# Head pairs whose scores are three fp32r products of halves: from the ninth pair on instead of the eleventh

## What is computed

```python
def _attn_ref(q, k, v, cap) -> np.ndarray:
    scale = 1.0 / np.sqrt(q.shape[-1])
    scores = scale * np.matmul(q, k.transpose(0, 1, 3, 2))
    scores = cap * np.tanh(scores / cap)
    ...
    attn = np.exp(scores)
    attn = attn / (np.sum(attn, axis=-1, keepdims=True) + 1e-09)
    return np.matmul(attn, v).astype(np.float32)

def _moe_ref(x, w_in, w_out, s, b) -> np.ndarray:
    h = x @ w_in
    r = np.maximum(h, 0.0)
    g = s * (r * r) + b
    return (g @ w_out).astype(np.float32)
```

## Time and profile before

| | |
|---|---|
| Median of 3 runs | 625.73 us (625.71 to 626.56) |
| The profiled execution's own time | 625.9 us |
| Span of the profile | 624.0 us |
| Busy PE, PEld, DVE, ACT, POOL | 617.2, 480.3, 330.9, 258.4, 46.3 us |
| Score products L352 (pairs 0 to 9) | 120 instructions, 64x448 |
| Score products L393 (pairs 10 to 23) | 252 instructions, 64x448 |
| Granted PE clock | 9 in all 40 slices of the page, mean 1.00 |

### The profile page before, as it was taken

The page is one execution under the profiler, slowest core; times in us unless marked ns, Lnnn a source line. Parts: engine busy times, 40 slices in busy tenths (PEclk is TensorE's granted clock), DMA queues, the critical chain, the costliest instruction groups (busy, mean ns, idle before and its releaser), DMA issues.

```text
span 624.0 us, 8174 instructions
## 1 busy us (share of the span) xinstructions
PE 617.2 (99%) x3206; PEld 480.3 (77%) x3206; DVE 330.9 (53%) x565; ACT 258.4 (41%) x272; POOL 46.3 (7%) x46
## 2 busy tenths in 40 slices
PE   7999999999999999999999999999999999999998
PEld 3335666777777777777779999999888888888997
DVE  4986999998677677677663332222411121111311
ACT  7885455656555555555413322222411121111220
POOL 0115724700000000000000000000000000000000
PEclk9999999999999999999999999999999999999999
DMA  8432245343222222231014112222522234111501
GB/s 289 143 117 61 87 155 157 108 130 94 72 92 87 76 88 91 71 92 58 29 60 148 59 51 58 70 78 75 175 79 59 66 112 125 48 42 33 165 2 64
DMA packets 31863, 57.17 MB, mean 92 GB/s; under 512 B 3536, under 2 KB 18000, under 8 KB 31824
## 3 DMA queue, kind: packets, MB, share of 16 engines
q1 hardware_dynamic: 31824, 56.64, 28.6%
HBM read 40.11 MB, written 16.52 MB: 91 GB/s over the span
## 4 chain that ended last, share of the span: by engine, by line
PE 95%; DVE 2%; DMA 1%; issue 1%; ACT 0%; SPq 0%; ACTq 0%; DVEq 0%
PE banks L480 13%; PE banks L482 13%; PE banks L481 13%; PE banks L497 12%; PE banks L496 12%; PE banks L498 12%; PE banks L438 8%; PE banks L393 5%; PE banks L352 3%; PE banks L450 2%; PE banks L418 1%; DMA work<-w_in 1%; PE banks L461 1%; DVE e_sum L725 0%; DVE w_lo L707 0%
## 5 line engine op out<-in xcount | busy, mean ns | idle before, releaser
L480 PE MATMUL banks<-x_hi,w_hi 128*128 128x448 f32 x384 | 142.9, 372 | 0.0
L482 PE MATMUL banks<-x_hi,w_lo 128*128 128x448 f32 x384 | 140.7, 366 | 0.0
L481 PE MATMUL banks<-x_lo,w_hi 128*128 128x448 f32 x384 | 140.6, 366 | 0.0
L497 PE MATMUL banks<-x_lo,w_hi 128*128 128x512 f32 (+2 forms) x384 | 139.4, 363 | 0.0
L498 PE MATMUL banks<-x_hi,w_lo 128*128 128x512 f32 (+2 forms) x384 | 139.4, 363 | 0.0
L496 PE MATMUL banks<-x_hi,w_hi 128*128 128x512 f32 (+2 forms) x384 | 139.4, 363 | 0.0
L813 DVE SCALAR_TENSOR_TENSOR x_lo<-e,beside,x_hi 128x512 fp32r<-128x512 f32 (+1 forms) x48 | 32.5, 683 | 115.5 <-ACT x_hi L641 115.5
L480 PEld LDWEIGHTS banks<-x_hi,w_hi 128*128 128x128 f32 x384 | 72.1, 188 | 15.0 <-issue 8.3
L641 ACT ACTIVATE x_hi<-e,beside 128x512 fp32r<-128x512 f32 (+1 forms) x48 | 31.7, 669 | 116.7 <-PE banks L498 116.7
L496 PEld LDWEIGHTS banks<-x_hi,w_hi 128*128 128x128 f32 x384 | 72.1, 188 | 9.0
L497 PEld LDWEIGHTS banks<-x_lo,w_hi 128*128 128x128 f32 x384 | 72.1, 188 | 8.9
(11 more groups left out here) (67 smaller groups left out, 550.0 us busy)
## 6 DMA issues: line engine op xcount, KB each, us to landing
hidden_scratch<-hidden_sb SPq DMA_DIRECT2D x48, 224.0 KB, 1.9
beside<-q_k SPq DMA_DIRECT2D x23, 448.0 KB, 4.0
e<-hidden_scratch SPq DMA_DIRECT2D x32, 256.0 KB, 2.7
e<-w_out SPq DMA_DIRECT2D x16, 384.0 KB, 3.1
work<-w_in SPq DMA_DIRECT2D x22, 256.0 KB, 5.5
v_sb<-v SPq DMA_DIRECT2D x24, 192.0 KB, 2.5
y_t<-beside SPq DMA_DIRECT2D x10, 256.0 KB, 2.1
e<-hidden_scratch SPq DMA_DIRECT2D x16, 160.0 KB, 2.2
```

What stands on the lines that cost most here:

```text
L480: nc.tensor.matmul(out, w_hi[:, j, w], x_hi[:, batch % 2, c, :], start=c == 0, stop=False)
L481: nc.tensor.matmul(out, w_hi[:, j, w], x_lo[:, batch % 2, c, :], start=False, stop=False)
L482: last = nc.tensor.matmul(out, w_lo[:, j, w], x_hi[:, batch % 2, c, :], start=False, stop=c == CT - 1)
L497: nc.tensor.matmul(out, w_hi[:, j, w], ring(x_lo, n), start=False, stop=False)
```

## The change

`SPLIT` goes from 2 * 6 - 2 = 10 to 6 + 2 = 8. Pairs 8 and 9 now take the split form.

```diff
-SPLIT = 2 * PAIRS - 2
+SPLIT = PAIRS + 2
```

## The result

The kernel after takes 627.45 us in the median of 15 runs (626.67 to 628.23), the kernel before, run beside it, 626.52 us (625.57 to 627.04). The ratio is 1.0018 with a 95% interval of 1.0011 to 1.0025: slower by 1.1 us, between 0.7 and 1.6. The forecast was 0.92 us more, the same sign and within the range. The executions shown ahead of the prediction (625.73 in the median) were among the shorter ones of before; over 15 runs its median is 626.5, so it is the forecast difference, 0.92, and not the forecast time of 626.65 that is held against the runs.

The account below looks back on a forecast made before the run. PE was taken to bound the kernel, with a DVE stretch without idle time delaying a load PE depends on. Terms -0.86, +0.77 and +1.01 gave +0.92 on 625.73, so 626.65 us; range 625.2 to 627.9 (8 in 10).

Parts of the forecast that it names:

- PE gains 0.86 us: Score blocks of pairs 8 and 9 on PE: the split form saves 0.43 us a pair, 0.86 us for two.
- The casts on ACT are free: Two new casts of 0.94 us fit ACT's idle time before tanh operations and cost nothing, 0.2 and 0.7 us to spare.
- First stall 0.77 us: PE at pair 8's first scores waits 0.77 us for the low half, whose DVE subtraction takes 2.18 us beside POOL.
- the later wait: PE's second stall, +1.01 us, at the tail scores of pairs 10 and 11, waiting for the tanh of pair 10.
- S = 1.55 us: S is the delay of DVE's square ahead of tile 5's store and pair 11's load; taken as 1.55, bounds 1.0 to 2.6.
- a walk through POOL's window: Stepping through DVE and POOL operations where they exclude each other; it cut the square's delay from 2.00 to 1.55 us.
- PE is later by S - 0.63: From the tail scores of pairs 10 and 11 on, PE lags by the square's delay less 0.63 us, whatever came earlier.
- Nothing behind the tail scores: After the tail scores of pairs 10 and 11 no further loss was counted: later loads are covered by ACT's and PE's slack.
- The term for the wait: At the tail scores of pairs 10 and 11, PE starts 0.1 us after the tanh it waits for ends.
- the sum: PE's total lateness at the tail scores of pairs 10 and 11: 1.55 - 0.63 = +0.92 us.
- The rival "slower": A square delay of 2.0 or more reaches pair 11's load, giving 627.1 to 627.7 us; slower from 1.88 on; chance 0.28.

Follow-up runs that it names:

- e6: Kernel after without the DVE subtractions for pairs 8 and 9, all their products reading the high halves; ratio to before 0.9998.
- e10: Kernel after with pair 8's cast and subtraction moved into idle time, q and k loads from pair 10 on one iteration earlier; ratio to before 0.9986.
- e3: Kernel after with only pair 8's cast and subtraction moved ahead into idle time of ACT and DVE; ratio to before 1.0005.
- e5: Kernel before plus two unused DVE subtractions where those for pairs 8 and 9 stand after the change; ratio to before 1.0021.
- e2: Kernel after with the q and k load of pair 11 moved ahead of the stores of tiles 4 and 5; ratio to before 1.0015.
- e4: Kernel after with pair 11's load ahead of the stores and pair 8's cast and subtraction moved into idle time; ratio to before 0.9998.
- e11: Kernel after with one more unused 128x448 DVE subtraction ahead of each of the subtractions for pairs 8 and 9; ratio to before 1.0038.

## Why the prediction was right, point by point

- **PE gains 0.86 us.** Right. e6 and e10 have 0.84 at the tail scores.
- **The casts on ACT are free.** Right as far as shown: e6 has both casts, and PE has no idle time up to the tail scores of pairs 10 and 11.
- **First stall 0.77 us.** Right in cause and size: 2.18 us for the subtraction as in the earlier trace rows, 0.73 us in the frame (75.84 against 75.11). That it is covered by the later wait is seen in e3 and e5, which have no first stall and lie on one line with after. With the late load gone it becomes a price of its own; e2 has it, e4 not.
- **S = 1.55 us, from 2.00 by a walk through POOL's window.** A little small. The square of tile 5 ended 1.70 late, the load was issued 1.68 late, and it landed after 5.2 us instead of the 5.0 of the earlier trace rows, so the tanh was 1.82 late. Against before, operations of DVE in POOL's window took more or less time: L729 +0.43, the first square +0.67, L752 +0.59, the copies of L755 and L765 -1.04 and -0.74, the last square -0.20. That is -0.29 on 2.00 where the walk had -0.45, so its order was right in the main; which of the two engines came first each time was a matter of tenths, and the prediction said so. The walk missed one operation, the `TENSOR_SCALAR` of L752 in front of the copies, which I had taken never to wait:

```profile
94.91 1.29 POOL L907 TENSOR_TENSOR w_lo<-work,w_hi 128x512 fp32r<-128x512 f32 x1
...
95.41 0.82 DVE L752 TENSOR_SCALAR quads<-parts,beside 32x28 f32<-32x28 f32 x1
```

  A quiet one takes 0.23 us. This one ended as POOL's operation did. The Trainium skill (SBUF — State Buffer, the list on what the engine side contends for) counts operations in a two-port mode among those that exclude POOL; if this one runs in such a mode, it has to wait, and the trace agrees with that.
- **PE is later by S - 0.63.** Right: S - 0.68 in four runs. The term for the wait, taken as 0.10, measured 0.05 (110.14 to 110.19).
- **Nothing behind the tail scores.** This term was wrong. From +1.14 at the tail scores the lateness grows to +1.61 at PE's last product: 0.05 in the tail block itself and 0.42 in three stretches of chunks in the long rhythm. Its reasons for later loads held in after: the next tail scores start at 138.90 and their tanh had ended at 138.19. The row of chunk 48 in the earlier trace rows and its neighbours showed one of the two rhythms, and I did not ask whether the other, at the same clock in the same trace, could come earlier. e10, in which PE waits nowhere in the loop, loses 0.28 of its 0.84 us in this way, so the long rhythm does not need a stall; and e5 shows that it does not need the new products.

So the 0.92 of the sum stand against 1.14 at its own place, and the remaining 0.47 are a term that the sum did not have. The two profiled executions differ by 1.61 in all, at the upper end of what the runs allow (0.7 to 1.6); that the runs' 1.1 lies so near to 0.92 is in part luck, as the missing term is in them too. The rival "slower" needed S of 1.88 or more at the square, where 1.70 was measured (1.82 at the tanh); the median ratio's 1.1 us lies just under the 1.25 us that divided it from the forecast, and its interval includes it.

## What to carry to other kernels

An engine with half its span idle can be the one that decides, if a stretch of the timeline shows it without idle time. Ask then for every operation put into that stretch not who reads its result but what stands behind it in every queue, DMA queues too; here it was the store ahead of a load. Where the gain is a tenth of a per cent, first give the new work a place in idle time and take the loads out from behind the stores: the same change, so placed, became a gain (0.9986).

## What the runs showed of the hardware that was not expected

A stream of fp32r products of 128x128 by 448 columns, each with new weights, runs with 202.7 or 206.7 ns from start to start at an unchanged granted clock of 1.00, and keeps one rhythm for whole stretches. In after, e2 and e11 it changed from long to short in the middle of a stretch, at chunk 48, where PE's program waits for POOL (0.27 and 0.22 us in e2 and e11, nothing to be seen in after). In e2 a stretch behind a wait of 0.32 us had the short rhythm, while in after and e5 the one behind the wait at 110 us had the long one, so a wait alone does not decide it. The Trainium skill (VectorE: DVE Perf Modes, the section on the trn2 errata) gives a matmul 6 cycles more than its columns. By that an estimate is 454 cycles, or 189 ns at 2.4 GHz; both measured rhythms are longer, and the formula has one value where the trace has two. What chooses the rhythm stays open.

Also open is the spread of executions: the two rhythms and the landing of the load (4.4 to 5.2 us for the same 448 KB) can each move the time by some tenths. That may be why the one profiled execution of e3 shows +0.77 where its runs show +0.3 (-0.3 to +0.9); no run shows it.
